# Moving half of the early weight sums of a Strassen-type second layer from beside attention into the end of the first layer

## The reference

```python
def phi(x):                                  # positive random features, 128 of them
    h = einsum('bhsd,md->bhsm', x, omega) - sum(x * x) / 2
    return exp(h - max(h)) / sqrt(128)
# q, k, v: (4 batches, 8 heads, 576 tokens, 64); q and k are scaled by 64 ** -0.25 first
kv, z = phi(k)^T v, sum over tokens of phi(k)
x = (phi(q) kv) / (phi(q) z + 1e-6)          # heads side by side: x is (2304, 512)
h = x @ w_in;  x = (h * clip(h + 3, 0, 6) / 6) @ w_out       # layer 1, d_ff 2048
h = x @ w2_in; out = (h * sigmoid(1.702 * h)) @ w2_out       # layer 2, d_ff 2048
```

## Time and profile before

| | |
|---|---|
| median of 3 runs | 890.46 us (890.45 to 890.55) |
| profiled execution | 890.09 us |
| its span, first to last instruction | 888.3 us |
| PE busy | 871.9 us, 98% |
| DVE busy | 616.6 us, 69% |
| ACT busy | 418.4 us, 47% |
| POOL busy | 233.0 us, 26% |
| mean DMA rate | 192 GB/s |
| granted clock, mean over the span | 0.995 |

### The profile page before, as it was taken

One profiled execution on the slowest core, in us unless ns is written; L12 is line 12 of the kernel. 1 busy time (PEld: TensorE's weight loads), 2 busy tenths in 40 slices (PEclk: granted clock), 3 DMA queues, 4 the chain that ended last, 5 costly groups with the idle time before them and its releaser, 6 DMA issues.

```text
span 888.3 us, 13924 instructions
## 1 busy us (share of the span) xinstructions
PE 871.9 (98%) x5029; PEld 787.7 (89%) x5029; DVE 616.6 (69%) x943; ACT 418.4 (47%) x858; POOL 233.0 (26%) x316
## 2 busy tenths in 40 slices
PE   8999999999999999999999899999999999999998
PEld 8988888778877888888887899999999999999998
DVE  6967786767658756675556547888747898477773
ACT  6856656544444545544445344335423355233432
POOL 2866565365655330032553410000000000000000
PEclk9999999999999999999999999999999999999999
DMA  9635554366564343117998946788998788887782
GB/s 277 186 105 144 133 163 98 85 148 168 132 166 103 84 94 68 28 37 202 284 274 246 316 140 213 255 257 258 274 309 252 262 255 261 291 277 249 253 260 75
DMA packets 186324, 170.54 MB, mean 192 GB/s; under 512 B 87824, under 2 KB 148368, under 8 KB 186256
## 3 DMA queue, kind: packets, MB, share of 16 engines
q1 hardware_dynamic: 164832, 167.00, 63.4%
q10 hardware_dynamic: 21424, 2.65, 2.1%
HBM read 128.52 MB, written 34.08 MB: 183 GB/s over the span
## 4 chain that ended last, share of the span: by engine, by line
PE 83%; DVE 6%; DMA 4%; SPq 3%; POOL 2%; ACT 1%; issue 1%; ACTq 0%; DVEq 0%; POOLq 0%
PE acc L1039 9%; PE acc L1041 9%; PE acc L1040 9%; PE acc L1097 5%; PE acc L1105 5%; PE acc L1104 5%; PE hid L1004 5%; PE hid L980 4%; PE hid L1005 4%; PE att L1041 4%; PE att L1039 4%; PE att L1040 4%; PE att L919 3%; PE att L882 2%; DMA combos<-X 2%; SPq L609 1%
## 5 line engine op out<-in xcount | busy, mean ns | idle before, releaser
L1097 PE MATMUL acc<-g_hi,w_out_hi 128*128 128x512 f32 x256 | 101.8, 398 | 4.0 <-DVE g_lo L1649 4.0
L1004 PE MATMUL hid<-x_hi,w_in_hi 128*128 128x512 f32 (+1 forms) x252 | 97.8, 388 | 2.4 <-DVE R L1644 2.4
L1105 PE MATMUL acc<-g_hi,w_out_lo 128*128 128x512 f32 x252 | 98.7, 392 | 0.0
L1104 PE MATMUL acc<-g_lo,w_out_hi 128*128 128x512 f32 x252 | 98.6, 391 | 0.0
L980 PE MATMUL hid<-x_lo,w_in_hi 128*128 128x512 f32 (+1 forms) x252 | 95.5, 379 | 0.6 <-DVE x_lo L1637 0.4
L1005 PE MATMUL hid<-x_hi,w_in_lo 128*128 128x512 f32 (+1 forms) x252 | 94.9, 377 | 0.0
L1336 ACT ACTIVATE g<-G 128x768 fp32r<-128x768 f32 x72 | 61.1, 848 | 70.7 <-PE acc L1041 38.1
L1688 DVE TENSOR_TENSOR g<-G,g 128x768 fp32r<-128x768 f32 x72 | 68.1, 955 | 24.9 <-ACT g L1336 24.9
L1644 DVE SCALAR_TENSOR_TENSOR R<-R,hid 128x512 f32<-128x512 f32 (+1 forms) x63 | 40.9, 649 | 57.3 <-ACT R L1259 57.2
L1259 ACT ACTIVATE R<-hid 128x512 f32<-128x512 f32 (+1 forms) x63 | 36.1, 572 | 94.5 <-PE hid L980 78.3
L1649 DVE TENSOR_TENSOR g_lo<-R,g_hi 128x512 fp32r<-128x512 f32 (+1 forms) x64 | 46.5, 727 | 26.8 <-ACT g_hi L1265 26.6
(11 more groups left out here) (278 smaller groups left out, 2264.4 us busy)
## 6 DMA issues: line engine op xcount, KB each, us to landing
ring_hi<-combos SPq DMA_DIRECT2D x134, 512.0 KB, 4.4
ring_lo<-combos SPq DMA_DIRECT2D x34, 512.0 KB, 4.4
combos<-stage SPq DMA_DIRECT2D x48, 256.0 KB, 2.9
combos<-stage SPq DMA_DIRECT2D x48, 192.0 KB, 2.6
stage<-w_raw SPq DMA_DIRECT2D x24, 256.0 KB, 3.3
out_t<-X SPq DMA_DIRECT2D x12, 384.0 KB, 6.0
X<-w_in SPq DMA_DIRECT2D x16, 256.0 KB, 3.1
X<-w_out SPq DMA_DIRECT2D x16, 256.0 KB, 3.3
```

The costliest lines, as they stand in the source:

```text
L1004: nc.tensor.matmul(bank, w_hi[0][:, at], x_hi[:, k, x0:x0 + t], start=(k == 0), stop=False)
L1097: nc.tensor.matmul(bank, w_hi[1][:, at], g_hi[:, g, 0:t], start=(s == 0), stop=False)
L1104: nc.tensor.matmul(bank, w_hi[1][:, at], g_lo[:, g, 0:t], start=False, stop=False)
L1105: last = nc.tensor.matmul(bank, w_lo[1][:, at], g_hi[:, g, 0:t], start=False, stop=(s == J - 1))
```

## The change

Four half-units in place of eight run beside attention, one every 8 half-steps from `g = 26` (loads at 26, 34, 42 and 50), each placed in POOL's queue right behind the squares of query rows; the four that stood behind key rows' squares are gone from there. The late ones are 28, from `g = 96`, one every 1.5 half-steps up to `u = 24`, then from `g = 128` one every 3 half-steps up to `u = 31`. Their high and low parts are now in two places: the plain quarters at `g + 3`, the sums one half-step later, the store at `g + 5` (from `u = 25` on all these are two half-steps later still). `x_first_sums` moves to `g = 150`, behind the sums of the last half-unit. Which of the four stage buffers a late half-unit uses follows from `u - EARLY_PREP`, as before. The work in all is the same but for this: the high and low parts of four half-units go from POOL to ACT and DVE.

```diff
-EARLY_PREP = 8
-LAST_PREP = 28
+EARLY_PREP = 4
+LAST_PREP = 25
...
         def prep_half(u):
             v = u - EARLY_PREP
-            return 26 + 4 * u if v < 0 else 6 * J + v * 8 // 5 if u < LAST_PREP else 8 * J + 4 * (u - LAST_PREP)
+            return 26 + 8 * u if v < 0 else 6 * J + v * 3 // 2 if u < LAST_PREP else 8 * J + 3 * (u - LAST_PREP)
...
+        def late_preps_at(half, late_by):
+            return [u for u in preps_at(half, late_by, late_by) if u >= EARLY_PREP]
...
-                for u in preps_at(g, 4, 4):
+                for u in preps_at(g, 4, 5):
                     store_combos(u)
...
-                if g == 2 * (LAST1 + 3):
+                if g == 2 * (LAST1 + 11):
                     x_first_sums()
...
-            def high_combos(u):
-                raw, sums_u, high, sums_high = stage(u)
+            def high_plain(u):
+                raw, _, high, _ = stage(u)
                 act.wait_ge(load_prep[stage_of(u)], 16 * uses_of(u))
                 nc.scalar.activation(high, raw[:, 0:3 * P], ACT.Copy).then_inc(prep_high, 1)
+
+            def high_sums(u):
+                _, sums_u, _, sums_high = stage(u)
                 act.wait_ge(prep_added, 4 * u + 4)
                 nc.scalar.activation(sums_high, sums_u, ACT.Copy).then_inc(prep_high, 1)
             def late_highs(half):
-                for u in preps_at(half, 3, 3):
-                    if u >= EARLY_PREP:
-                        high_combos(u)
+                for u in late_preps_at(half, 4):
+                    high_sums(u)
+                for u in late_preps_at(half, 3):
+                    high_plain(u)
...
-            def low_combos(u):
-                raw, sums_u, high, sums_high = stage(u)
+            def low_plain(u):
+                raw, _, high, _ = stage(u)
                 dve.wait_ge(prep_high, 2 * u + 1)
                 dve.wait_ge(prep_added, 4 * u + 4)
                 nc.vector.tensor_tensor(raw[:, 0:3 * P].bitcast(F32R), raw[:, 0:3 * P], high.bitcast(F32), ALU.subtract).then_inc(prep_low, 1)
+
+            def low_sums(u):
+                _, sums_u, _, sums_high = stage(u)
                 dve.wait_ge(prep_high, 2 * u + 2)
                 nc.vector.tensor_tensor(sums_u.bitcast(F32R), sums_u, sums_high.bitcast(F32), ALU.subtract).then_inc(prep_low, 1)
             def late_lows(half):
-                for u in preps_at(half, 3, 3):
-                    if u >= EARLY_PREP:
-                        low_combos(u)
+                for u in late_preps_at(half, 4):
+                    low_sums(u)
+                for u in late_preps_at(half, 3):
+                    low_plain(u)
```

## The result

The changed kernel takes 893.01 us (median of 7 runs, 891.19 to 893.57) against 890.45 us for the kernel before (7 runs): a ratio of 1.0033, with a 95% interval of 1.0022 to 1.0044. It is 0.33% slower where 0.8% faster was forecast, and it lies outside the range. The profiled execution has a span of 891.5 us, 3.2 us more than before. Lines of the kernel after stand 4 lines lower up to `x_first_sums` and 8 lower in the DVE code (L1649 is now L1657).

A forecast was written before the change was run, and what follows sets the result against it. PE, busy 98% of the span, was taken as the bound, so only its stalls and low-clock time could be won. Terms 2.4 + 1.3 + 0.8 + 2.5 = 7.0 us off 890.46 forecast 883.4 us, range 880.9 to 887.6.

The forecast's parts named there:

- Attention: Stalls at 197, 256 and 284 in layer 1's attention should go, 3.7 us forecast in all.
- 483 and 488: End of chunk 3: stall of 1.34 shrinks to 0.9, stall of 0.36 goes; 0.8 us gained, bounds -0.5 and 1.7.
- the stall at 504: Chunk 4: moving the x sums away wins stall and low clock, 3.9 us, less 1.2 and 0.2: 2.5 us.
- Stalls at 197 and 256: Attention: query rows no longer wait behind a store's landing in SP's queue, so both stalls go: 2.4 us.
- Chunk end at 284: Second chunk end: POOL's squares end earlier, DVE's four low parts of x shorten from 4.41 to 2.76 us: 1.3 us.
- The stall of 1.37 at the first chunk end stays: First chunk end, at 163: stall and low clock behind it unchanged, as everything ahead is the same in both kernels.
- Hidden, with 1 to 2 us to spare: I put zero: Late layer 1: the split's longer buffer wait, 9.9 us of work within 13.6 us (2 less for some places), costs nothing.
- The pair's cycle: SP's stores, landing wait and loads for a pair of late half-units: 7.2 us, with 8.2 us available.
- the lock: At 504, POOL's x sums and DVE's two-SBUF-input low parts share a port pair; the second blocks until the first finishes.
- the 1.2 forecast: Chunk 4, at about 518: moved x sums meet DVE's low parts of `u = 31`, stalling PE 0.6 to 1.8 us.
- the stores set the pace: Rival, 8%: slower stores and landings make pairs of late half-units late, stalls and clock falls follow: 892.2 us.
- The late stall only moves: Rival, 20%: in chunk 4 both x sums hold DVE in one step, PE stalls 2.2, clock falls again: 886.2 us.

The follow-up runs named there:

- one place: Changed kernel with a late half-unit's high and low parts together again and its stores one half-step earlier: 891.74 us, 1.0024.
- x sums last alone: Kernel before with POOL's two x sums behind the last half-unit's sums and waiting for DVE's last low parts: 887.05 us, 0.9965.
- ring late alone: Changed kernel with the first ten loads of layer 2's ring moved back to half-steps 150 to 158, nothing else: 891.16 us, 1.0015.
- evacuation first: Changed kernel with chunk 3's evacuation ahead of the odd half's parts in step 64, on ACT and DVE: 892.77 us, 1.0025.
- evacuation first and ring late: Changed kernel with chunk 3's evacuation ahead of step 64's odd-half parts and layer 2's first ten ring loads at half-steps 150 to 158: 885.62 us, 0.9966.

## Why the prediction was wrong

The stalls and falls of the clock put a price on each term. Attention won 2.4 us of the 3.7 forecast. At 483 and 488 a gain of 0.8 was forecast, and 3.5 were lost (0.9 won; 2.7 of stall and 1.7 of low clock lost). For the stall at 504 a gain of 2.5 was forecast, and 1.0 was lost (3.9 won; 2.27 and 0.94 of stalls and 1.7 of low clock lost). So of the 9.6 us between forecast and result 4.3 lie at the end of chunk 3, 3.5 in chunk 4 and 1.3 in attention; the last 0.5 is within the scatter of the lead-in.

- *Stalls at 197 and 256 (2.4 forecast)*: this term failed too. The wait was found rightly: the query rows go out at 178.01 with no store's landing ahead of them, and DVE no longer waits for POOL's rows. But 0.50, 0.65 and 0.72 us are left, 0.6 us less in this pair of profiles, and even that is scatter: from the start of `gate(19)` to that of `gate(31)` the four kernels with the old early places take 88.1 to 89.1 us, and the nine with the new ones 88.4 to 90.0. In the trace of the changed kernel DVE's two-input instructions are held by POOL's work on the half-unit (bias 1.04 us for 0.17 at 190.46), its transposes end at 193.46, and ACT issues q_phi's block moves (2.60 us) ahead of the gate that PE waits for. That chain is read from the profile; the run without early half-units has only one of the stalls (0.30), which says that they come from this work, not which link matters. The prediction named one wait and forgot that the work stayed.
- *Chunk end at 284 (1.3)*: right in its cause, too small. The four low parts take 2.50 us, against 4.41, and the stall is gone. From `gate(31)` to `gate(34)` it is 2.3 to 2.7 us less, so the place gave about twice the stall of 1.28 that the profile lists; where the rest comes from stays open.
- *"The stall of 1.37 at the first chunk end stays"*: right for this change, and the largest thing passed over. The same reading as at 284, squares and low parts at one time, stood in the trace at 156 (four low parts of 5.04 us) and would have shown 3.8 us to be had by one number.
- *483 and 488 (0.8)*: half right. 1.34 fell to 0.48, as forecast (0.9 was the size given to it); the stall at 488 grew by 2.7 and brought a fall of the clock. The step that failed is the next one.
- *"Hidden, with 1 to 2 us to spare: I put zero"*: this is the step that failed first and cost most. That it was the store cycle is shown by one place, where the load goes out 5.9 us earlier and the stall of 3.03 is 0.36. The pair's cycle was put at 7.2 us and measured 8.55, against the 8.16 it had. Two terms were small. From the first store of a pair to the start of its last there were 4.2 - 0.5 = 3.7 us forecast, and it takes 435.92 - 431.27 = 4.65, since single issues grow to 0.8 and 1.0 us on fuller engines; the landing was put at the median 2.9 of the earlier trace rows and takes 3.7 there (3.5 at the median of the new kernel, 2.5 to 5.0). With 0.4 for the load that makes 4.65 + 3.7 + 0.4 = 8.75 in the round shown. A slack of 1 us out of 8 that rests on medians of a lighter load was none.
- *The stall at 504 (2.5)*: the lock was right, the 3.9 us won were near (x sums last alone gives 3.0), and 0.94 for the 1.2 forecast was right with luck, as ring late alone and its 2.29 show. But the price of the traffic was not seen, the second step that failed: `u = 26` to `u = 31` were given 0.2 us, and with raw landings of 5.2 us at the median and 8.1 at most they cost 2.27 and a fall of the clock. The prediction did count chunk 3's GB/s and not chunk 4's, where the ring's loads stand between seven half-units and not four.
- *Rivals*: "the stores set the pace" (8%, 892.2) came nearest to the 893.0. Its mechanism is what happened up to 488; its size there was 2.7 us of delay for 7 forecast, with the traffic of chunk 4 making up the rest. Its threshold, a landing of 3.9 us, was passed at 3.5 because the stores had grown as well. "The late stall only moves" (20%) is not what the changed kernel did: there the x sums cost 0.94 us and the stall of 2.27 comes from a late load. Ring late alone did pay what that rival feared, 2.29 us and a fall of the clock.

What stays open: whether the late side of the changed kernel really gains when the early ones move (3.6 us in one pair of profiles, 0.7 by the medians; no run separates it), and which link keeps the stall of 0.7 us at 193.

The best version tried is 1.1% faster than the kernel before: four early half-units behind the first chunk end, ring late, evacuation first (0.989).

## What to carry to other kernels

When work moves into a stretch, recompute the round trip of each buffer with the traffic that the move itself makes: issue, landing and the order in the queue all grow, and a slack of a tenth made from medians is no slack. Look for the same pattern (one engine's long instructions beside another's) at every place of the trace, also where the change does nothing: the best gain here was one chunk end away. And try a sound part of a change by itself: two of its parts pay alone, the sum did not.

## What the runs showed of the hardware

- In chunk 4 a raw load lands in 3.1 to 3.9 us with the ring's loads kept away (evacuation first and ring late), at DMA shares of 1.07 and 0.95 in 16 us each, and in 3.9 to 8.1 us with them between (the changed kernel), at 1.05, 0.93 and 1.11. The share alone does not tell the two apart; what else is queued does.
- A DMA instruction on SP mostly takes 0.35 to 0.9 us in the changed kernel, and now and then 1.9 to 2.9 us in its chunk 4, where the DMA share is 0.93 to 1.11.
- Beside POOL's x sums of 1.9 to 2.1 us, DVE instructions with two SBUF inputs that start behind them take 2.0 to 2.3 us in place of 0.4 to 0.7; a product that reads PSUM keeps its 0.41.
- The clock fell to 1.2 GHz for 3.4 us at a time (in some cases 6.8) in or right behind stalls of 1.0 to 6.2 us, but not with each: the same 0.99 at 163 had it in the changed kernel's profile and not in those of one place and ring late, and one place had 2.01 us at 508, and the run in which the x sums wait 2.99 at 488, without it. The fall is to be counted as a chance, not as a price that comes with a length of stall.
